# Products with w_out taken block by block, two blocks behind the products with u

## The reference

```
def _moe2_ref(x, w_in, w_out):      # x (2304, 512), w_in (512, 2048), w_out (2048, 512)
    h = x @ w_in
    g = h - np.tanh(h)
    return (g @ w_out).astype(np.float32)
```

## Time and profile before

| | |
|---|---|
| time, median of 3 runs | 1024.71 us (1023.49 to 1026.56) |
| profiled execution, its own time | 1024.66 us |
| span of its trace | 1022.6 us |
| TensorE busy | 887.1 us, 87% |
| VectorE, ScalarE, GpSimd busy | 544.5, 549.6, 294.2 us |
| last stage | from 780.2 us of the span to its end |

### The profile page before, as it was taken

The page is one execution under the profiler, slowest core; times in us unless marked ns, Lnnn a source line. Parts: engine busy times, 40 slices in busy tenths (PEclk is TensorE's granted clock), DMA queues, the critical chain, the costliest instruction groups (busy, mean ns, idle before and its releaser), DMA issues. The chain is left out here.

```text
span 1022.6 us, 16577 instructions
## 1 busy us (share of the span) xinstructions
PE 887.1 (87%) x5707; PEld 661.6 (65%) x5707; DVE 544.5 (53%) x1031; ACT 549.6 (54%) x855; POOL 294.2 (29%) x207
## 2 busy tenths in 40 slices
PE   3898998998998998998999997977565699999998
PEld 3766666666667766666666665543122488888887
DVE  4566456456555565565565565240005966776671
ACT  2656566566566566565566565111004866666660
POOL 4353333233234134135135100000000333344341
PEclk9999999999999999999999999788877799999999
DMA  3402202202202102102012000558972200000000
GB/s 115 133 24 70 70 2 70 69 0 69 69 1 69 55 15 69 42 27 69 26 43 69 16 9 2 203 208 307 398 282 76 90 21 22 29 21 21 21 21 31
DMA packets 48864, 75.49 MB, mean 74 GB/s; under 512 B 5056, under 2 KB 23488, under 8 KB 48320
## 3 DMA queue, kind: packets, MB, share of 16 engines
q1 hardware_dynamic: 48832, 75.06, 21.6%
HBM read 70.32 MB, written 4.72 MB: 73 GB/s over the span
## 5 line engine op out<-in xcount | busy, mean ns | idle before, releaser
L474 DVE TENSOR_REDUCE part_neg<-ps 128x1 f32<-128x384 f32 x432 | 222.3, 552 | 104.5 <-PE ps L301 95.4
L531 ACT ACTIVATE probT<-ps 128x384 f32<-128x384 f32 x288 | 141.2, 490 | 178.8 <-PE ps L318 178.2
L518 ACT ACTIVATE prob<-ps,neg_max 128x1152 f32<-128x1152 f32 x144 | 175.4, 1218 | 60.1 <-DVE neg_max L477 60.1
L318 PE MATMUL ps<-ident,prob 128*128 128x128 f32 x1296 | 169.9, 276 | 36.4 <-ACT prob L518 36.2
L301 PE MATMUL ps<-kT,qT_hi 128*128 128x384 f32 x480 | 175.1, 381 | 14.2 <-DVE probT L408 8.6
L318 PEld LDWEIGHTS ps<-ident,prob 128*128 128x128 f32 x1296 | 143.0, 141 | 58.2 <-issue 29.2
L334 PE MATMUL ps<-probT,v_nat 128*64 128x320 f32 (+1 forms) x1152 | 155.2, 415 | 0.3 <-ACT probT L531 0.3
L301 PE MATMUL ps<-kT,qT_lo 128*128 128x384 f32 x480 | 155.0, 339 | 0.0
L408 DVE COPY probT<-ps 128x384 f32<-128x384 f32 x128 | 70.8, 553 | 103.3 <-PE ps L318 101.0
L1064 POOL TENSOR_TENSOR g_lo<-g,g_hi 128x1024 fp32r<-128x1024 f32 x36 | 86.5, 2403 | 134.9 <-ACT g_hi L1034 134.9
L301 PEld LDWEIGHTS ps<-kT,qT_hi 128*128 128x128 f32 x480 | 89.3, 189 | 53.6 <-DVE probT L408 27.5
(11 more groups left out here) (142 smaller groups left out, 987.9 us busy)
## 6 DMA issues: line engine op xcount, KB each, us to landing
ring<-in_moe_w SPq DMA_DIRECT2D x10, 2048.0 KB, 20.0
k_nat<-in_k SPq DMA_DIRECT2D x16, 576.0 KB, 4.0
v_nat<-in_v SPq DMA_DIRECT2D x16, 576.0 KB, 5.2
q_nat<-in_q SPq DMA_DIRECT2D x32, 256.0 KB, 4.5
w_first<-in_moe_w SPq DMA_DIRECT2D x4, 2048.0 KB, 13.7
out<-res SPq DMA_DIRECT2D x18, 256.0 KB, 2.0
x<-in_moe_w SPq DMA_DIRECT2D x2, 2048.0 KB, 11.3
x<-in_moe_w_in SPq DMA_DIRECT2D x1, 4096.0 KB, 29.5
```

The costliest lines, as they stand in the source:

```text
L318: last = nc.tensor.transpose(chunk_bank(s, c)[:, n * P:(n + 1) * P], src[:, kt * P:(kt + 1) * P], ident[:])
L474: nc.vector.reduce_max(part_neg[:, c:c + 1], slot_banks(s)[:, c, 0:CW], AX.X, negate=True).then_inc(part_done, 1)
L518: nc.scalar.activation(prob[prob_index(par, n)][:].rearrange("p (b c) -> p b c", b=NCH), slot_banks(s)[:, :, 0:CW], ACT.Exp, bias=neg_max[ ...
L531: evac_chunk(lambda d, s_: nc.scalar.activation(d, s_, ACT.Copy), s, j, c).then_inc(side_evac, 1)
```

## The change

The portions of `project` become blocks: for block b both groups take its four tiles, 12 matmuls for each group. `project` of block b follows `hidden` two blocks on (`LAG = 2`): chunk 0's first two blocks run behind its own `hidden` 2 and 3, and after the loop 48 matmuls are left, not 96. Both accumulators are open through four portions, and both are ended in the portion of block 3. ScalarE makes `g_hi` of the block before ahead of `big`, not behind it. VectorE copies both accumulators after block 1 of the next chunk. Each group's wait for `o_evac` stands before its part of block 0.

```
-            def project(c, par, n0, n1):
-                for n in range(n0, n1):
-                    i, ft = divmod(n, FT)
-                    t = c * TPC + i
-                    if ft == 0:
+            def project(c, par, b):
+                pe.wait_ge(gl_done, c * BLOCKS + b + 1)
+                pe.wait_ge(gh_done, c * BLOCKS + b + 1)
+                for i in range(TPC):
+                    if b == 0:
                         wait(pe, o_evac[i], c)
-                    if i == 0 and ft % FB == 0:
-                        pe.wait_ge(gl_done, c * BLOCKS + ft // FB + 1)
-                        pe.wait_ge(gh_done, c * BLOCKS + ft // FB + 1)
-                    if i == 0 and ft % PF == 0:
-                        pe.wait_ge(wl_done, ft // PF + 1)
-                    for k, (a, w) in enumerate(((g_hi, w_hi), (g_hi, w_lo), (g_lo, w_hi))):
...
+                    for ft in range(b * FB, (b + 1) * FB):
+                        if i == 0 and ft % PF == 0:
+                            pe.wait_ge(wl_done, ft // PF + 1)
+                        for k, (a, w) in enumerate(((g_hi, w_hi), (g_hi, w_lo), (g_lo, w_hi))):
...
+                    if b == BLOCKS - 1:
                         last.then_inc(o_full, 1)
...
             def body(c, par):
                 for b in range(BLOCKS):
                     hidden(c, b)
-                    if not is_first(c):
-                        project(c - 1, par ^ 1, b * per, (b + 1) * per)
+                    if b >= LAG:
+                        project(c, par, b - LAG)
+                    elif not is_first(c):
+                        project(c - 1, par ^ 1, b - LAG + BLOCKS)
             over_chunks(pe, body)
-            project(CHUNKS - 1, (CHUNKS - 1) % 2, 0, TPC * FT)
+            for b in range(BLOCKS - LAG, BLOCKS):
+                project(CHUNKS - 1, (CHUNKS - 1) % 2, b)
...
                     nc.scalar.activation(th, h_of(b), ACT.Tanh, scale=-1.0).then_inc(th_done, 1)
-                    act.wait_ge(sq_done, m + 1)
-                    nc.scalar.activation(big[b % 2][:], sq[b % 2][:], ACT.Relu, bias=edge[:]).then_inc(big_done, 1)
                     if b:
                         high(c, par, b - 1)
                     elif not is_first(c):
                         high(c - 1, par ^ 1, BLOCKS - 1)
+                    act.wait_ge(sq_done, m + 1)
+                    nc.scalar.activation(big[b % 2][:], sq[b % 2][:], ACT.Relu, bias=edge[:]).then_inc(big_done, 1)
...
-                        for i in range(TPC):
-                            if ((i + 1) * FT - 1) // (TPC * FT // BLOCKS) == b:
+                        if b == LAG - 1:
+                            for i in range(TPC):
                                 evac(c - 1, i)
```

More of the change, by code:

```diff
@@ L909, in mlp @@
     PF = FT // PIECES
+    LAG = 2
     with ExitStack() as ctx:
@@ L993, in hidden @@
                 last.then_inc(h_full, 1)
-            def project(c, par, n0, n1):
-                for n in range(n0, n1):
-                    i, ft = divmod(n, FT)
-                    t = c * TPC + i
-                    if ft == 0:
-                        wait(pe, o_evac[i], c)
-                    if i == 0 and ft % FB == 0:
-                        pe.wait_ge(gl_done, c * BLOCKS + ft // FB + 1)
-                        pe.wait_ge(gh_done, c * BLOCKS + ft // FB + 1)
-                    if i == 0 and ft % PF == 0:
-                        pe.wait_ge(wl_done, ft // PF + 1)
-                    for k, (a, w) in enumerate(((g_hi, w_hi), (g_hi, w_lo), (g_lo, w_hi))):
-                        last = nc.tensor.matmul(ps[:, 2 * HB + i, :], a[par][:, ft, i * P:(i + 1) * P], w[:, ft, :],
-                                                start=(ft == 0 and k == 0), stop=(ft == FT - 1 and k == 2))
-                    if ft == FT - 1:
+            def project(c, par, b):
[3 more added lines that the diff above has]
+                    if b == 0:
+                        wait(pe, o_evac[i], c)
+                    for ft in range(b * FB, (b + 1) * FB):
+                        if i == 0 and ft % PF == 0:
+                            pe.wait_ge(wl_done, ft // PF + 1)
+                        for k, (a, w) in enumerate(((g_hi, w_hi), (g_hi, w_lo), (g_lo, w_hi))):
+                            last = nc.tensor.matmul(ps[:, 2 * HB + i, :], a[par][:, ft, i * P:(i + 1) * P], w[:, ft, :],
+                                                    start=(ft == 0 and k == 0), stop=(ft == FT - 1 and k == 2))
+                    if b == BLOCKS - 1:
                         last.then_inc(o_full, 1)
-            per = TPC * FT // BLOCKS
             def body(c, par):
```

## The result

The changed kernel took 1028.63 us in the median of 10 runs (1026.65 to 1031.96), the kernel before 1023.5 us in 10 (1019.23 to 1026.56). The ratio is 1.0052, with a 95% interval of 1.0034 to 1.0069: slower by half a per cent. The forecast was 1026.7 us in a range of 1021.5 to 1033.5. The range held. By the prediction's own border of 0.3% the result is "slower", to which it had given 0.395, and not "the same", which had 0.55. Single executions of the kernel before spread over 7 us here, not over the microsecond that is called ordinary at the start of this text; what decides is the interval of the ratio.

The account below looks back on a forecast made before the run. The prediction took TensorE alone to set the pace from 814.80 us on. Accumulator waits of +12.4 us, +0.3 in the last chunk and -10.7 at the start gave +2.0 us: 1026.7 us, stated range 1021.5 to 1033.5.

Parts of the forecast that it names:

- border of 0.3%: Whole kernel: a measured difference up to about 0.3%, 3.1 us, cannot be told from no change.
- gain at the start: Start of the last stage: earlier portions fill TensorE's idle time, putting its end 10.7 us ahead.
- 7 x 1.65: Last stage, chunks after the first paying one: TensorE waits 1.65 us in each of seven for group 0's accumulator copy.
- layout of the block: One steady block timed from its `hidden`: group 0's copy ends at +7.89, TensorE's next weight load not before +7.95.
- The tail's 0.3: Last chunk, with no `hidden` between two portions: TensorE waits 0.3 us for `g_lo`, once.
- wait of 0.8 us for block 2: Chunk 0, start of the stage: TensorE waits about 0.8 us before block 2's portion, already counted in block 3's start.
- What was predicted for `w_lo`: GpSimd in the start: with `g_lo` earlier, `w_lo` pairs fall clear of its subtraction; 1.21 us each, previously up to 1.635.
- `g_lo`'s hand-over: Steady blocks: `g_lo` ends at +6.07, TensorE wants it at +6.3; fits with 0.2 us, no cost taken.
- (a): TensorE's clock falls to half level in each of eight accumulator waits: +15 us, 1041.6 us; chance 0.09.
- (b): VectorE's copy with `big` and GpSimd's `g_lo` hold each other up in each block: 1046 us; chance 0.04.
- (c): `g_lo` reaches TensorE 0.5 us late in most blocks: +4.5 us, 1031 us; chance 0.08.
- (d): Accumulators between chunks cost nothing because the copy comes in time: 1014.3 us; chance 0.04.

Follow-up runs that it names:

- kernel with the early copy: Changed kernel with VectorE's copy of group 0's accumulator moved between the series and the copy of tanh of block 1: 1014.52 us, ratio 0.9907 to the kernel before.
- second profile of the change: The changed kernel timed and profiled once more with no edit: 1028.6 us, ratio 1.0038 to the kernel before.

## Why the prediction came out as it did

**The mechanism was right.** The gain at the start is given back at the accumulators, chunk by chunk. The kernel with the early copy shows both by themselves: without the waits the end was predicted at 1009.0 us of the span, 228.7 after the stage's start, and measured at 229.5; the waits for the copies are the 13.7 us between it and the changed kernel.

**The size was off by 2 us.** The sum was +2.0, the second profile of the change has +4.1 (243.2 against 239.1), and the medians say +3.4 and +5.1. The term mis-sized is "7 x 1.65", which is 7 x 1.81 in the profile. The layout of the block was right up to the copy's end, +7.89 predicted and +7.90 measured. From there to TensorE's weight load the prediction had 0.06 us; it is 0.22. The prediction had said that some latency in this wait stands in no row, and its range for the wait, 1.35 to 1.95, does take in 1.81; only the middle was too low. It makes 1.1 us, and 0.2 more come with the first wait (0.82 + 0.24 us, predicted 0.85). The start is the other half: chunk 0's block 3 came 0.4 us later than predicted, and the work from there, without the waits, took 0.6 us more (195.2 us in the kernel with the early copy, not 194.6), 0.3 of it in that first portion. The tail's 0.3 did not come (the last 48 matmuls follow after 0.03 us). In all 1.3 + 1.0 - 0.3 = 2.0 of the 2.1 us. With a forecast 2.0 us over, and the border at 3.1, such a sum decides between "same" and "slower"; that is where the word went wrong.

**Two errors in the start did not count.** The first portion, at half clock for most of its length, took 7.9 us in the second profile (793.23 to 801.17) and not 7.1, and the wait of 0.8 us for block 2 all but vanished (0.16 us in the first profile). Neither moved block 3, whose start `g_lo` sets. What was predicted for `w_lo` held: with `g_lo` earlier none takes over 1.23 us, and with `big` first, in the changed kernel, one takes 1.64 again.

**The parts that cost nothing.** The portion put before `hidden` 3 costs nothing: TensorE has no wait that goes back to it, with the loads or without. `g_lo`'s hand-over held with its 0.2 us of slack (it ends at +6.08, and the weight load would be at +6.30): no wait for it in a steady block. Group 1's copy and the two stores close together cost no wait in either profile of the change.

**The rivals.** (a), the clock, did not happen: behind waits of 1.56 to 1.59 us never, 28 of them in four profiles. It was not far: behind those of 2.16 to 2.19 us it came in five of seven. (b), VectorE and GpSimd: the copy of tanh started inside `g_lo` and took 1.36 us. The Trainium skill, SBUF — State Buffer, "SBUF: two separate sides", confines the lock to instructions with two SBUF inputs or a two-port mode; the trace agrees. (c): no late `g_lo` with the change's order; with `big` first it came as described, at half of what exceeds the slack. (d) is out for this kernel, and is what one moved copy makes of it (1014.3 us predicted, 1014.52 measured). The two ratios of the same kernel, 1.0052 and 1.0038, lie within each other's intervals; how often a load is late, as in the first profile, was not measured.

## What to carry to other kernels

Accumulators that are left open over a whole chunk must all be emptied between two neighbouring portions: before a loop is interleaved by blocks, lay out one round with the measured distances and ask where the copy comes in its engine's queue. More accumulators would be the other way, but this kernel's eight PSUM banks are all in use (four for the products with u, two for tanh, two accumulators). The mend can be a slot where that engine waits anyway, here 0.8 us between two elementwise instructions, which turned +0.5% into -0.9%. And price a wait of TensorE whole: here the idle time in the waits' view is 1.57 us and the loss 1.81, and between the end of the copy and the first weight load lie 0.22 us, which a sum of durations leaves out.

## What the runs showed of the hardware

The clock does not answer to the length of a wait alone. After waits of 1.56 to 1.59 us, 28 in four profiles, it stayed at 2.4 GHz each time; after 2.16 to 2.19 us, in one profile, it fell to 1.2 GHz five times and stayed twice; after 2.04 and 2.64 us, in another, it fell from the third and the fourth matmul on. After 1.56 and 1.74 us in the start (the changed kernel and the one before with `g_hi` first) it stayed up; after 3.68 us, at the place of the 1.56, it fell. A wait only 0.6 us longer so cost 12 us over the kernel, where its own length in all is 4.8.
